# Loading the second head pair's keys and queries in ten parts among the bias steps

## What is computed

```python
scores = scale * q @ k^T
psi_rel = log1p(abs(i - j));  psi_i = log1p(max(i, 1))
x = psi_rel / psi_i                      # one number per (i, j)
bias = relu(x * w1 + b1) @ w2            # 32 hidden units, 8 heads
attn = softmax(scores + bias)
x = attn @ v                             # laid out as tokens of 512
...                                      # gates choose one of 8 experts per token
out = p[e] * (relu(x @ w1[e]) @ w2[e])   # 512 -> 1024 -> 512
```

## Time and profile before

| | us |
|---|---|
| median of 3 runs | 704.93 (704.23 to 705.63) |
| profiled execution, its own time | 702.18 |
| its span | 700.5 |
| PE busy | 651.3 (93%) |
| DVE busy | 377.3 (54%) |
| ACT busy | 345.2 (49%) |
| POOL busy | 195.3 (28%) |

### The profile page before, as it was taken

One profiled execution on the slowest core, in us unless ns is written; L12 is line 12 of the kernel. 1 busy time (PEld: TensorE's weight loads), 2 busy tenths in 40 slices (PEclk: granted clock), 3 DMA queues, 4 the chain that ended last, 5 costly groups with the idle time before them and its releaser, 6 DMA issues. The chain is left out here.

```text
span 700.5 us, 14223 instructions
## 1 busy us (share of the span) xinstructions
PE 651.3 (93%) x4353; PEld 520.5 (74%) x4353; DVE 377.3 (54%) x803; ACT 345.2 (49%) x727; POOL 195.3 (28%) x178
## 2 busy tenths in 40 slices
PE   6777899999999999999947899999999999999994
PEld 3223788888888888888636788888888888888883
DVE  5999666666666666666376452477415422221220
ACT  4997656666666666666420432476324422221221
POOL 4000624444444444448301111112111111111101
PEclk9999999999999999999955999999999999999998
DMA  7777625448544545551374841338011111011100
GB/s 170 202 195 205 125 46 110 102 109 218 125 100 104 111 95 114 111 108 36 129 265 133 304 151 45 115 136 325 31 45 45 37 45 44 30 45 45 45 0 1
DMA packets 67961, 77.06 MB, mean 110 GB/s; under 512 B 46543, under 2 KB 47055, under 8 KB 67920
## 3 DMA queue, kind: packets, MB, share of 16 engines
q1 hardware_dynamic: 63392, 64.58, 35.0%
q0 software_dynamic: 4144, 11.54, 5.0%
q10 hardware_dynamic: 384, 0.44, 0.2%
HBM read 69.06 MB, written 11.27 MB: 115 GB/s over the span
## 5 line engine op out<-in xcount | busy, mean ns | idle before, releaser
L610 ACT ACTIVATE sm<-sm,negmax 128x576 f32<-128x576 f32 x144 | 111.3, 776 | 6.3 <-DVE negmax L799 4.5
L799 DVE CUSTOM_DVE_ANT_0 sm<-ps_s,bias 128x576 f32<-128x576 f32 x128 | 91.6, 753 | 28.1 <-PE ps_s L1084 28.1
L822 DVE COPY pT<-ps_t 128x512 f32<-128x512 f32 x80 | 55.1, 689 | 70.2 <-PE ps_t L1107 70.2
L1008 DVE TENSOR_TENSOR hTlo<-ps_s,hThi 128x512 fp32r<-128x512 f32 x50 | 32.2, 686 | 92.7 <-ACT hThi L733 92.6
L1270 PE MATMUL ps_pv<-w2hi,hThi 128*128 128x512 f32 x200 | 80.5, 402 | 1.4 <-DVEq L988 1.4
L1270 PE MATMUL ps_pv<-w2hi,hTlo 128*128 128x512 f32 x200 | 78.3, 391 | 0.0
L1270 PE MATMUL ps_pv<-w2lo,hThi 128*128 128x512 f32 x200 | 77.9, 390 | 0.0
L1247 PE MATMUL ps_s<-w1hi,xThi 128*128 128x512 f32 x200 | 64.6, 404 | 5.4 <-DVE xTlo L980 3.6
L725 ACT ACTIVATE hsb<-ps_s 128x512 f32<-128x512 f32 x25 | 15.0, 599 | 110.1 <-PE ps_s L1247 104.1
L1159 PE MATMUL ps_pv<-pT,vt 128*64 128x320 f32 (+1 forms) x512 | 69.1, 412 | 0.0
L558 POOL DMA_INDIRECT out_dram<-ysb,sidx x25 | 25.5, 1020 | 156.5 <-ACT ysb L740 156.5
(11 more groups left out here) (184 smaller groups left out, 1264.4 us busy)
## 6 DMA issues: line engine op xcount, KB each, us to landing
w1raw<-in_moe_w_dram SPq DMA_DIRECT2D x18, 1024.0 KB
w2raw<-in_moe_w_dram SPq DMA_DIRECT2D x18, 1024.0 KB
raw<-in_kq_dram SPq DMA_DIRECT2D x32, 432.0 KB, 5.3
bias<-stage SPq DMA_DIRECT2D x32, 288.0 KB, 3.2
raw<-in_kq_dram SPq DMA_DIRECT2D x32, 128.0 KB, 4.9
vt<-in_v_dram SPq DMA_DIRECT2D x32, 128.0 KB, 2.4
tokens_dram<-xl SPq DMA_DIRECT2D x64, 64.0 KB, 1.7
bias_tail<-stage SPq DMA_DIRECT2D x4, 144.0 KB, 2.4
```

The lines of the kernel that those rows point to most:

```text
L610: nc.scalar.activation(probs, probs, ACT.Exp, scale=-1.0, bias=negmax[:, u % 2, hd:hd + 1], accum_out=sums[:, pr % 2, 2 * t + hd:2 * t + h ...
L799: nc.vector.tensor_tensor_reduce(sm[:, u % 2, S * hd:S * (hd + 1)].rearrange("p (a c) -> p a c", a=2), ps_s[:, hd, :, 0:HALF], bias.rearra ...
L822: nc.vector.tensor_copy(dst, src).then_inc(copied_a, 1)
L1008: V.tensor_tensor(hTlo[:, 4 * i:4 * i + 4, :].rearrange("p k t -> p (k t)"), ps_s[:, 1, i, :], hThi[:, 4 * i:4 * i + 4, :].bitcast(F32).re ...
```

## The change

The six transfers of `load_qk(1)` no longer stand behind the last bias step. Pair 1's keys and queries are loaded by ten transfers instead, five for each half of the partitions: the 442 KB transfer is cut into three of 147 KB, the other two stay. One of the ten is issued behind the transfer of each bias step `m` = 25 to 34 (of 0 to 35). POOL's wait for the data of pair 1, and so that of all odd pairs, counts ten transfers for pair 1 and six for each later one. `load_v(1)` and `load_qk(2)` move up in SP's queue by the six transfers taken out ahead of them.

```diff
+FINE = 5
...
+            def load_second_pair(i):
+
+                half, part = divmod(i, FINE)
+                rows = slice(D * half, D * (half + 1))
+                if part < 3:
+                    nc.sync.dma_start(raw[rows, 1, part, :], kq[0, 1][:, part, :]).then_inc(raw_in[1], 16)
+                else:
+                    load_qk_part(1, half, part - 2)
+
...
                     nc.sync.dma_start(bias_tail[odd, :, P * FULL:S], stage[1::2, k, 0:TAIL]).then_inc(bias_stored[k], 16)
-            load_qk(1)
+                if m >= STEPS - 1 - 2 * FINE and m < STEPS - 1:
+                    load_second_pair(m - (STEPS - 1 - 2 * FINE))
             load_v(1)
...
             def split_pair(pr):
                 s = pr % 2
-                pool.wait_ge(raw_in[s], 96 * (pr // 2 + 1))
+                pool.wait_ge(raw_in[s], 32 * (PARTS * (pr // 2 + 1 - s) + FINE * s))
```

## The result

| kernel | median us (range, runs) | ratio to before [95%] |
|---|---|---|
| before, all its runs at that time | 703.36 (702.08 to 705.63, 8) | 1 |
| changed | 699.31 (698.30 to 703.23, 8) | 0.9944 [0.9927, 0.9962] |
| changed, timed again | 698.82 (696.76 to 701.66, 6) | 0.9930 [0.9907, 0.9952] |

The change makes the kernel faster by 4.05 us. Two things add up in that. With more runs the kernel before came out at 703.36 instead of 704.93, so the base was 1.6 us too high; and the gain was 4.05 us, where 3.1 had been reckoned. (The second timing has its own runs of before beside it, with a median of 703.71.)

A forecast was written before the change was run, and what follows sets the result against it. The prediction took the pair 0 to pair 1 seam, where PE waits for POOL's split, as the place to win: -4.87 + 1.65 + 0.1 = -3.1 us, off 704.93, gives 701.8 us; range 699.7 to 703.9.

The forecast's parts named there:

- The bound: Seam between pairs 0 and 1: 21.96 us against 17.09, so no edit there can win more than 4.87 us.
- Part 1: Seam: the load comes earlier, POOL splits pair 1 in time, and PE's pause goes, -2.78 us.
- Part 2: Seam: without the pause PE's slow clock behind it goes, with the waits behind it, -2.09 us.
- rival 2: Near 86 us: the clock falls all the same behind the new DVE stall, up to 1.7 us more; chance 0.1.
- Part 3: Bias stage: its steps carry the load, backlog 1.9 us against ACT's 2.07 free; cost 0 to 0.2, taken as 0.1 us.
- The upper bound: Bias stage: pricing the parts by pair 3's whole load, 8.55 us, gives a backlog of 4.65 and a loss of 2.6 us.
- Part 4: Behind the seam: pair 2's load moves up, POOL's second split stalls DVE's denominators 1.68 us, costing +1.65 us.
- rival 1: Seam: second split starts 0.9 us or more later, denominators slip past POOL; gain 4.0 to 4.9 us, some 700.5; chance 0.2.
- the other bound: Denominators at the seam: a loss of 2.65 us if DVE meets the start of one of POOL's operations.
- Rivals 3 to 5: Rival 3: bias-stage parts cost Part 3's upper bound, 704.3, chance 0.1; rival 4: own line; rival 5: change does nothing, chance 0.05.
- rival 4: Bias stage: stores land so late that ACT paces it; slower, net +2.6 us, 707.5; chance 0.05.

The follow-up runs named there:

- Spread and held: Against the changed kernel: the ten parts behind every second bias step, over twenty steps, and pair 2's split held until pair 0's denominators are made; ratio 0.9920.

## Why the prediction was right and where it failed

**The bound** held. The best seam is 17.09 us, so no more than 4.87 could be won there, and 4.7 to 4.9 is what the executions without a meeting win on it.

**Part 1** (the pause, -2.78): right in all four traces, but not by its dates. The first split began 39.9 to 40.3 us behind the 15th slot write, where 36.1 was forecast (69.2 - 33.11): some 4 us late. The margin to PE is 0.1 to 0.5 us, where I had written 4, so that the pause went by luck more than by the room that I had reckoned with. By its own bound, "a first split later than 73.2" was a sign of being wrong, and so were ACT's waits for transfers and stores landing after more than 5.3 us (up to 7.6); all three came, the first in three traces of four. In the profiled execution PE's time for the first scores had moved from 80.88 to 81.49 as well, and that saved it.

**Part 2** (the clock, -2.09): right in three traces of four. In the fourth the slow stretch came back behind the new pause, as rival 2 said, at its price of 1.7 us.

**Part 3** (the load in the bias stage) is **the step that failed**. I took the engines' share as additive: stores leave 0.26 of each step free, and the parts need 5.8 us at the load's own rate of 204 GB/s, so a backlog of 1.9 us. But 0.74 busy at 195 GB/s and 0.96 at 204 do not add up in this way. Mixed, they moved 213 GB/s at a share of 1.03, 212 with the parts spread, and 225 at the most with every third step. What was asked for was 195 + 1.18 MB / 15.1 us = 273 GB/s. By these numbers I estimate the backlog at (273 - 213) x 15.1 us = 0.9 MB, or 4.3 us at that rate: 2.4 more than I had. What it did can be read: the last part was issued at 66.12 instead of 64.8 and landed 7.3 us later, where I had reckoned with 4.4. In the same way ACT's 2.07 us of freedom are exceeded by 2.2, and it waited 2.6 us. That the term in the sum was nearly right (0.1 forecast; 0.2 to 0.4 measured on the way to pair 0's last scores) was luck, owed to a cover that I had not named: DVE's split of pair 0, which lets ACT finish 1.8 us late almost for nothing. The upper bound, 2.6 us of loss, was the nearer reading for ACT and the wrong one for PE.

The Trainium skill, page "DMA: Bandwidth & Descriptors", section "Rules for kernel authors", asks to coalesce. The runs here do not bear it out for pieces of 147 KB: behind the last step the cut load comes to 0.9963 [0.9946, 0.9980] of the whole one, and among the stores it is 0.9944 [0.9927, 0.9962] of before for the cut load and 1.0001 [0.9979, 1.0023] for the whole one, which was also asked for within fewer steps. The section "Anatomy of one DMA" of the same page of the Trainium skill, which I had cited for a fixed 2 us in every transfer, gives that figure for transfers issued by GpSimd, while SP issues these. The last of ten parts behind the last step landed at 75.6 us, the last of six whole transfers at 75.9, so no such part adds up here from one transfer to the next.

**Part 4** (the stall, +1.65) followed it into error, and it is the term by which the sum was off. Pair 2's load stands behind ACT's late last slot write and the same backlog: its first transfer was issued at 71.28 instead of 68.6, its six took 6.2 to 7.1 us to land where 5.2 had been reckoned, and its data were there at 81.8, not at 77 to 78. So the second split ran not ahead of pair 1's first scores but 0.4 to 0.9 us behind them, and the denominators met its third operation or nothing, never the middle of the fourth. That is **rival 1**, to which I gave 0.2, and it names this condition ("0.9 us or more later than I reckon"). It was true in three traces of four, with a stall of 0 to 0.2 us, though by another way than I wrote: DVE did not come into the third operation's rest but just ahead of its start. In the fourth it was the other bound: not 1.65 but 2.5 of stall, 2.2 of PE's wait and 1.7 of clock, 3.9 us. I had priced the stall and the clock in different cases; in three of the four traces in which such a meeting made PE wait some 2 us, they came together. Weighing the four traces of the changed kernel, (3 x 0.1 + 3.9) / 4 = 1.05 us, against the 1.65 in my sum.

**The sum:** -4.87 + 1.05 + 0.35 = -3.5 us for a mean over such executions, and -4.4 for one without a meeting. The medians give -4.05 and, timed again, -4.9. The direction and the size of the gain were about right; that four traces with one meeting in them stand for the runs is an assumption. A range that reached to rival 1 was right, but it hung on a median of three runs that was 1.6 us too high.

**Rivals 3 to 5:** the parts did not cost the upper bound on PE's path, the bias stage was not paced as a whole (rival 4 needed whole transfers), and the change does what it says.

The best version is the changed kernel with the second split held, 698.05 us, with parts close together: 0.9928 [0.9906, 0.9950]. It can't be told from the changed kernel's own 0.9930 [0.9907, 0.9952] by time, only by the traces. Spread and held, 0.9920 [0.9902, 0.9937], can't be told from it either, and its stretches are 0.7 us longer, so that I would not prefer it.

## What to carry to other kernels

Before a load is put among other transfers, compare the bytes asked for with the rate of the mixture, not the free share of one with the rate of the other alone; and if someone waits for the transfers beside it, ask for the load in small pieces spread over several steps. When POOL's long operations move in time, look at every short DVE instruction that they can now meet; if they need not run just then, hold them behind it with one wait, which costs nothing and takes the chance out. Where the trace shows a margin of tenths of a microsecond, one profiled execution is one throw of the dice: take several, and compare stretches rather than spans.

## What the runs showed of the hardware

- Which of two instructions started first, by 0.03 us, decided over 2.5 us: behind POOL's start DVE's 0.16 us instruction took 2.64 us (84.26 against 84.23), 0.15 us ahead of it 0.16 us. The Trainium skill, page "SBUF — State Buffer", section "Who interferes with whom", says that the one that issues first keeps the port for its whole instruction. All seven traces agree: where the denominators were slow, they ended within 0.04 us of POOL's operation.
- A single wait of PE of 1.9 to 2.7 us at this seam was followed by a stretch at half clock in seven traces of eight (2.66, 2.54, 2.46, 2.19, 2.17, 2.08 and 1.88 us), at a cost of some 1.7 us more. The eighth is the kernel with ten parts behind the last step: a wait of 2.10 us, and full clock from 83 to 93 us. It and the kernel before with the held split, whose wait was 1.39 us, had been at half clock before that, in pair 0 (from 69.2 to 72.6 and from 70.5 to 73.9). Why is open.
- In the last 16 us of the bias stage the stores from SBUF to SBUF ran alone at 193 to 195 GB/s with a share of 0.74, and together with a load into 64 partitions at 208 to 225 GB/s with a share of about 1: where the stores had left a quarter of the engines' time free, the mixture moved only 15 to 30 GB/s more.
- With no stores beside them, transfers of up to 147 KB landed after 3.4 us in the median and those of up to 442 KB after 5.3, so ten small ones were in no later than six large ones. Among the stores the small ones took 6.2 us.
- The same program without a meeting ran in 694.3 and in 699.3 us of span, and 3.4 us of the difference were two stretches in which the clock had been granted differently, over 270 us behind the edit.
